# Moving a two-axis Fourier transform into the attention stage: feature axis first, chunk by chunk, and one batch's transforms beside the other batch's work

## The reference, cut to what matters

```python
# stage 1: blockwise linear attention with a decay per head
for b in range(nb):
    intra = einsum('bhic,bhjc->bhij', qb, kb) * Dmask      # lower triangle, lam**(i-j)
    out[:, :, sl] = intra @ vb + (qb * lam_pow) @ kv_state
    kv_state = lam_block * kv_state + (kb * rev_pow).T @ vb
# stage 2: Fourier mixing, layer norm, a wide MLP
u = x + real(fft(fft(x, axis=1), axis=2))                  # axis 1: tokens, axis 2: features
un = (u - mean(u)) / sqrt(var(u) + 1e-6)
x = u + relu(un @ w_ch1) @ w_ch2                           # 512 -> 2048 -> 512
# stage 3: causal convolution over 5 tokens as a gate
gate = sigmoid(sum_k conv_w[k] * x shifted)
out = (gate * (x @ w_val)) @ w_out
```

## Time and profile before

| | us |
|---|---|
| median of 3 runs | 487.25 (487.1 to 487.63) |
| the profiled execution, its own time | 487.47 |
| its span | 485.7 |
| busy: PE, DVE, POOL, ACT | 453.2, 245.2, 169.1, 135.7 |

### The profile page before, as it was taken

How to read it: one execution, slowest core, us unless ns; L and a number is a source line. 1 busy time by engine, 2 the same in 40 slices (tenths; PEclk the granted TensorE clock), 3 DMA queues, 4 the chain that set the end, 5 groups by cost and what they waited for, 6 DMA issues and landing times.

```text
span 485.7 us, 6750 instructions
## 1 busy us (share of the span) xinstructions
PE 453.2 (93%) x2700; PEld 435.9 (90%) x2700; DVE 245.2 (50%) x342; ACT 135.7 (28%) x240; POOL 169.1 (35%) x107
## 2 busy tenths in 40 slices
PE   6999998297979999999999999999999999399997
PEld 5999997296869999999999999999999999399885
DVE  2334758948986132753212321322262899799110
ACT  1252435020543106211022211112123524434221
POOL 1341978546496300520003300013106309235320
PEclk9699999598989999999999999999999999699999
DMA  7997300000202200130000220001400000001112
GB/s 227 363 372 239 103 1 0 1 1 0 87 0 88 86 1 0 43 131 1 1 0 2 86 86 0 0 0 33 142 0 1 1 1 0 0 1 65 66 43 87
DMA packets 12009, 28.69 MB, mean 59 GB/s; under 512 B 1352, under 2 KB 3024, under 8 KB 11984
## 3 DMA queue, kind: packets, MB, share of 16 engines
q1 hardware_dynamic: 11984, 28.34, 16.8%
HBM read 25.18 MB, written 3.15 MB: 58 GB/s over the span
## 4 chain that ended last, share of the span: by engine, by line
PE 76%; DVE 17%; DMA 2%; issue 2%; POOL 1%; ACT 1%; DVEq 0%
PE ps L692 8%; PE ps L693 8%; PE ps L691 8%; PE ps L669 8%; PE ps L667 8%; PE ps L668 8%; DVE xT L1145 5%; PE ps L535 5%; PE ps L507 2%; PE ps L756 2%; PE ps L757 2%; PE ps L755 2%; PE ps L518 2%; PE ps L734 2%; PE ps L735 2%; PE ps L736 2%
## 5 line engine op out<-in xcount | busy, mean ns | idle before, releaser
L1088 DVE SCALAR_TENSOR_TENSOR hl<-ps,hh 128x384 fp32r<-128x384 f32 x64 | 34.9, 555 | 123.8 <-ACT hh L842 123.6
L842 ACT ACTIVATE hh<-ps 128x384 fp32r<-128x384 f32 x64 | 31.3, 490 | 169.3 <-PE ps L669 169.3
L1228 POOL TENSOR_TENSOR w1l_a<-raw_a,w1h_a 128x1024 fp32r<-128x1024 f32 x4 | 10.0, 2498 | 120.5 <-ACT w1h_a L798 120.5
L1145 DVE SCALAR_TENSOR_TENSOR xT<-u_pad,cw,xT 128x768 f32<-128x768 f32 x32 | 44.6, 1460 | 6.0 <-ACT xT L869 6.0
L691 PE MATMUL ps<-hh,w2h_a 128*128 128x384 f32 x128 | 45.1, 352 | 0.0
L667 PE MATMUL ps<-cen_h,w1h_a 128*128 128x384 f32 x128 | 43.5, 340 | 0.2 <-issue 0.2
L692 PE MATMUL ps<-hl,w2h_a 128*128 128x384 f32 x128 | 43.4, 339 | 0.0
L693 PE MATMUL ps<-hh,w2l_a 128*128 128x384 f32 x128 | 43.4, 339 | 0.0
L669 PE MATMUL ps<-cen_h,w1l_a 128*128 128x384 f32 x128 | 43.3, 338 | 0.0
L691 PE MATMUL ps<-hh,w2h_b 128*128 128x384 f32 x128 | 43.2, 338 | 0.0
L693 PE MATMUL ps<-hh,w2l_b 128*128 128x384 f32 x128 | 43.2, 338 | 0.0
(11 more groups left out here) (167 smaller groups left out, 1028.1 us busy)
## 6 DMA issues: line engine op xcount, KB each, us to landing
chunks<-in_qkv SPq DMA_DIRECT2D x12, 512.0 KB, 5.8
chunks<-in_qkv SPq DMA_DIRECT2D x24, 256.0 KB, 6.8
raw_a<-in_mlp SPq DMA_DIRECT2D x8, 512.0 KB, 4.6
raw_b<-in_mlp SPq DMA_DIRECT2D x8, 512.0 KB, 4.5
out<-out_sb SPq DMA_DIRECT2D x12, 256.0 KB, 2.0
raw_a<-in_val SPq DMA_DIRECT2D x2, 512.0 KB, 4.4
raw_b<-in_out SPq DMA_DIRECT2D x2, 512.0 KB, 4.2
seq_c<-const_seq SPq DMA_DIRECT2D x1, 642.0 KB, 11.7
```

The costliest lines, as they stand in the source:

```text
L842: nc.scalar.activation(hh[:, slot, j], ps[2 * slot + j][:, 0:TB], ACT.Relu).then_inc(s_hh, 1)
L1088: stt(hl[:, slot, j], ps[2 * slot + j][:, 0:TB], 0.0, hh[:, slot, j].bitcast(F32), ALU.max, ALU.subtract).then_inc(s_hl, 1)
L1145: stt(xT[:, b, r], u_pad[:, b, r, PAD - d:PAD - d + S], cw[:, K - 1 - d, r:r + 1], xT[:, b, r], ALU.mult, ALU.add).then_inc(s_tap, 1)
```

## The change: what it does, and its diff

- **Attention output.** The values are now stationary and the masked scores moving, so the output comes out transposed and goes straight to `xT`: no transposes, no identity, no `x_tok`. A product has 64 stationary columns and writes the lower or the upper half of the partitions. The state product is likewise eight products of 64 x 64 instead of four of 128 x 128.
- **Banks.** The scores have two banks instead of four, so `scores(n+1)` waits until both masks of chunk n are done. The hidden blocks of the MLP have two banks instead of four as well: `hidden(n+1)` waits for `hidden_lo(n)`.
- **Transforms.** The feature axis comes first, per chunk: `radix4` on DVE (four instructions), `hid_transform` on PE, five copies on ACT. Then the radix-6 stage over the chunks of a batch on DVE (`chunk_pair`, `two_pairs`, `third_pair`: 514 columns an instruction, 16 instructions a batch), `mirror` on ACT, and `seq_tile` on PE: twelve products with at most 128 moving columns for each of four feature tiles. `add_u` now has eight DVE instructions a tile instead of four.
- **Placing.** Batch 0's radix-6 stage and tiles stand in batch 1's attention. Batch 1's stand in the first steps of the MLP on batch 0, whose step order is changed for that.
- **Memory and transfers.** The chunk buffers are a ring of three: the load of chunk n waits for the attention of chunk n-3.
- **Tail.** `x3_lo` (four instructions) and `gate_lo` (sixteen) move from POOL to DVE.

```diff
-        START_ORDER = [(0, 0), (1, 0), (2, 0), (2, 1), (3, 0), (3, 1), (0, 1), (1, 1)]
+        START_ORDER = [(0, 0), (1, 0), (0, 1), (1, 1), (2, 0), (2, 1), (3, 0), (3, 1)]
...
+            def from_chunk(n):
+                for hp in range(HP):
+                    for par in range(2):
+                        m = mm(out_bank(n)[par * Dh:(par + 1) * Dh, hp * P:(hp + 1) * P], vr[c][:, 2 * hp + par, :],
+                               probs[:, n % 2, 2 * hp + par, :], start=n % NC == 0 and hp == 0, stop=True,
+                               skip_group_check=True)
...
+            def hid_transform(n):
+                for i in range(2):
+                    mm(bank[:, cols], z[:, i], hid_c[:, cols], start=True, stop=True)
+                mm(bank[:, 2 * P:4 * P], z[:, 2], hid_c[:, 2 * P:4 * P], start=True, stop=False)
+                mm(bank[:, 2 * P:4 * P], z[:, 3], hid_c[:, 4 * P:6 * P], start=False, stop=True).then_inc(s_hy, 1)
...
+            def seq_tile(b, a):
+                t = b * R + a
+                if a == 0:
+                    pe.wait_ge(s_r6, R6 * (b + 1))
+                for im, bank in ((0, ps[COS]), (1, ps[SIN])):
+                    if t:
+                        pe.wait_ge(s_u, UA * (t - 1) + (UA if im else UA // 2))
+                    for g, (re_row, im_row) in enumerate(((4, 5), (1, 2))):
+                        mm(o, spectrum(b, re_row, im, a), seq_c[:, at:at + P], start=True, stop=False)
+                        mm(o, spectrum(b, im_row, im, a), seq_c[:, at + P:at + 2 * P], start=False, stop=True)
...
+            for n in range(N):
+                if n + 1 < N:
+                    scores(n + 1)
+                if n % NC < NC - 1:
+                    state_product(n)
+                if n % NC:
+                    from_state(n)
+                if n >= 1:
+                    hid_transform(n - 1)
+                from_chunk(n)
+                if NC + 1 <= n < NC + 1 + R:
+                    seq_tile(0, n - NC - 1)
+            hid_transform(N - 1)
             mean(0)
-            hid_transform(1, 2)
-
             mlp_hidden(first_steps[0])
-            mlp_hidden(first_steps[1])
-            mean(1)
 
             def mlp_step(st, after):
+                if after and st.n != 3:
+                    mlp_hidden(after)
+                if st.n == 1:
+                    seq_tile(1, 1)
+                if st.n == 2:
+                    seq_tile(1, 3)
+                mlp_out(st)
                 if st.n == 0:
+                    seq_tile(1, 0)
+                if st.n == 1:
+                    seq_tile(1, 2)
+                if st.n == 3:
+                    mean(1)
+                    mlp_hidden(after)
...
+            def third_pair(b):
+                chunk_pair(b, 2)
+                tt(y[:, 0], y[:, 0], sd[:, 2], ALU.add).then_inc(s_r6, 1)
+                tt(y[:, 2], sd[:, 1], sd[:, 2], ALU.subtract).then_inc(s_r6, 1)
+                tt(y[:, 5], sd[:, 4], sd[:, 5], ALU.add).then_inc(s_r6, 1)
...
             def mlp_step(st, after):
-                if after and st.n > 1:
+                if st.n == 3:
+                    add_mlp(st)
+                    for hf in range(2):
+                        centre(1, hf)
+                        cen_lo(1, hf)
+                if after:
                     hidden_lo(after)
-                add_mlp(st)
+                if st.n in (1, 2):
+                    add_u(1, 2 * (st.n - 1))
+                if st.n != 3:
+                    add_mlp(st)
                 if st.n == 0:
-                    centre(1, 1, (0,))
+                    third_pair(1)
+                if st.n in (1, 2):
+                    add_u(1, 2 * st.n - 1)
...
+                if st.n == M_LAST + 3:
+                    x3_lo(0)
                 if st.n in (M_LAST + 4, M_LAST + 6):
                     taps(0, st.n - M_LAST - 4)
+                if st.n in (M_LAST + 5, M_LAST + 6):
+                    x3_lo(st.n - M_LAST - 4)
```

More of the change, by code:

```diff
@@ L38, in fourier_constants, with hid, seq @@
     p = np.arange(P)[:, None]
[L39 to L43, removed]
+    R, G = D // P, S // P
+    def hid(k):
+        th = 2 * np.pi * ((p * k[None, :]) % D) / D
+        return np.cos(th), np.sin(th)
+    n = np.arange(P // 2)
+    c0, s0 = hid(R * n)
+    im0 = -s0
+    im0[:, :1] = hid(np.array([D // 2]))[0]
+    c2, s2 = hid(R * n + 2)
+    odd = 2 * np.arange(P) + 1
+    co, so = hid(odd)
+    turn = np.where(odd % R == 1, 1.0, -1.0)[None, :]
+    hid_tab = np.concatenate([c0, im0, c2, -s2, co, -so, -so * turn, -co * turn], 1).astype(np.float32)
+    def seq(g, count):
+        th = 2 * np.pi * ((p * (G * np.arange(count)[None, :] + g)) % S) / S
         return np.cos(th), np.sin(th)
@@ L174, in program @@
+        with ExitStack() as second_l:
+            cen_l1 = sb_in(second_l, "cen_l1", [P, R, S], F32R)
+        mirrored = sd[:, :, 0:D].rearrange("p g (i k) -> p g i k", i=2)
+        sb("region3_rest", [P, NC * YW])
         raw = [raw_a, raw_b]
@@ L760, in _ @@
             value(0)
-            for tb in range(NB):
-                if tb + 1 < NB:
-                    value(tb + 1)
-                project(tb)
+            value(1)
+            project(0)
+            value(2)
+            project(1)
+            value(3)
+            project(2)
+            project(3)
         @block.scalar
@@ L1172, in mlp_step @@
                     taps(0, st.n - M_LAST - 4)
+                if st.n in (M_LAST + 5, M_LAST + 6):
+                    x3_lo(st.n - M_LAST - 4)
             each_step(dve, mlp_step)
             finish_mlp(3, nc.vector, dve)
-            for r in range(R):
-                gated(0, r)
+            gated(0)
+            gate_lo(0)
+            x3_lo(3)
             taps(1, 0)
-            for r in range(R):
-                gated(1, r)
+            gated(1)
+            gate_lo(1)
             taps(1, 2)
@@ L1182, in _ @@
             for tb in (2, 3):
-                for r in range(R):
-                    gated(tb, r)
+                gated(tb)
+                gate_lo(tb)
         @block.gpsimd
@@ L1289, in _ @@
             split_lo(AFTER_G, value_splits())
-            x3_lo(0)
-            x3_lo(1)
-            x3_lo(2)
             split_lo(AFTER_V, out_splits())
-            gate_lo(0)
-            x3_lo(3)
-            for tb in range(1, NB):
-                gate_lo(tb)
 def kernel(**inputs):
```

793 lines of the change are left out of this document (327 added, 466 removed).

## The result

The changed kernel takes 498.76 us (median of 4 runs, 496.85 to 504.38) against 487.18 in the runs beside it: 1.023 times the time before, 95% interval 1.018 to 1.028. The prediction said 498.5. The time is right, and the mechanism is right in the main: PE gains in the attention and loses more than that in waits for DVE inside the MLP's first steps.

The account below looks back on a forecast made before the run. PE was taken to bound attention and MLP, DVE the transforms and tail. Hidden(31) ending 9.2 us later (attention gain, MLP waits, clock) and 1.8 of tail gave 487.5 + 9.2 + 1.8 = 498.5 us; range 488 to 508.

Parts of the forecast that it names:

- The chunk: Attention on PE: a chunk's five parts, transposes gone and feature transform added, take 4.98 us instead of 5.27.
- The column-half rival: Attention's chunk part: column halves take turns instead of overlapping, 0.97 us more a chunk, 505.5 us in all; chance 0.20.
- The ring of three: Chunk loads: the ring starves PE, 9 chunks by up to 0.8 us, 7 us, 505.5 us in all; chance 0.05.
- First tile of batch 0: In batch 1's attention: PE waits 5.1 us for third_pair(0), which ends at 62.1; the tile ends at 64.8.
- T: End of three turns of 4.98 + 2.65 + 0.3 us after batch 0's first tile: 88.5 us.
- The MLP's first steps: Batch 1's tiles (10.6 us) and PE's waits (19.6 us) stand inside the MLP, the longest wait 6.9 us at third_pair(1).
- The clock: Clock falls behind PE's waits of over 3 us ahead of the MLP's steady part: 3 x 2.0 = 6 us, bounds 0 and 14.
- newton: MLP step 7: newton(0) and newton(1) together on DVE make hidden_lo(9) late for hidden(10) by 1.4 us, bounds 0 and 3.
- The tail: Behind hidden(31): x3_lo on DVE ahead of gated(0), less 2.1 us of collision, 0.3 for waits: 1.8 us more.
- 1.14 us a tap alone: Tail on DVE: price of a tap without POOL working, against 2.1 us beside POOL; taps(0, 2) takes 12.8 instead of 14.92.
- The signs: Trace signs: PE idle ahead of tiles, clock 0.5 behind, hidden(5) near 181 us, L436 about 1.1, DVE busier, POOL less.
- DVE undisturbed: Rival: none of the charged DVE collisions with POOL happens, gaining 13.9 us, 484.6 us in all; chance 0.14.

Follow-up runs that it names:

- the third experiment: Against the changed kernel, the four x3_lo and sixteen gate_lo go back from DVE to POOL; 502.1 us, ratio 1.032 to the kernel before.
- fourth experiments: Against the changed kernel, hidden blocks from step 5 on use four banks in turns of two; 498.23 us, ratio 1.024 to the kernel before.
- the filled waits: Against the changed kernel, PE multiplies ones into a free bank in five waits for DVE; 497.03 us, ratio 1.021 to the kernel before.
- the first experiment: Against the changed kernel, each feature tile of batch 1 stands one MLP block later in PE's list; 485.92 us, ratio 0.998 to the kernel before.

## Why the prediction was right, and where not

- **The chunk** (4.98 us forecast, 5.13 measured). State product 0.6 and 0.61, feature transform 1.30 and 1.31, chunk's part 1.1 and 1.02. What was missed is 0.20 us on the state's part, 1.09 instead of 0.89. It now stands behind the 64-column products, and its operands have changed places (the state is stationary), which the prediction did not count among the changes. Once, behind the full-array products of a tile, the same eight records take 0.94 us from end to end (91.92 to 92.86):

```profile
91.53 0.39 PE L476 MATMUL ps<-seq_c,sd 128*128 128x64 f32 x2
91.75 1.11 PE L425 MATMUL ps<-qd,state 128*128 128x128 f32 x8
```

So most of the 0.20 us comes with the change of shape. The Trainium skill, TensorEngine Tiling (Array Packing), section Key Properties, says that a change of tiling mode drains the engine; the extra time behind the change of shape agrees.
- **The column-half rival** fell: the halves overlap. The ring of three cost no wait in mid-stream that matters (in this profile PE waited for `chunks` once, 1.29 us at the start; in others it waited up to 0.99 us ahead of `scores(8)` in turn 7, and at most 1.3 us in all, where the rival had 7), so that rival fell too.
- **First tile of batch 0**: forecast at 62.1 after a wait of 5.1 us, measured at 61.46 after 2.93; PE came later, since the products behind the wait of 3.35 us ran at a granted clock of 0.61. **T**, the end of the last tile turn: 88.5 forecast; the last tile of batch 0 ended at 91.7; the tile behind the first wait took 5.3 us at 1.2 GHz instead of 2.65.
- **The MLP's first steps**: third_pair's wait 6.9 forecast, 5.48 measured; the others 2.7, 2.2, 2.6, 0.6 and 3.7 forecast, 2.75, 2.31, 2.74, 0.84 and 3.07 measured. Here the step failed that put the first variance among the work of out(0) at no cost: the epsilon waits behind `two_pairs(1)`, 3.47 us. Since 1.4 of that shortens the next wait, the term was 2.1 us too small.
- **The clock** (6 us, bounds 0 and 14): 10.8 in the profiled execution, 7.5 and 7.7 in those of the third and fourth experiments. In the median it is about 5, an estimate: 10.8 less 5.6, if all of the profiled execution's excess is the clock's. The size stood within its bounds and near its value; the filled waits show the mechanism, not the median's size.
- **newton** (1.4 us): 1.40 measured.
- **The tail** (+1.8 us) had the wrong sign. From the last relu of hidden(31) to `gated(0)` on PE it was 24.36 us and is 22.77 (415.33 to 438.10), so -1.6. The step that failed is "1.14 us a tap alone": the 9.13 us for eight taps in the earlier trace rows had a POOL `x3_lo` beside them for 1.8 us (381.86 to 385.38), whose row was not among those read:

```profile
381.86 3.52 POOL L1253 TENSOR_TENSOR cen_l<-u_pad,cen_h 128x1536 fp32r<-128x1536 f32 x1 [5.02 <-ACT cen_h L861]
```

Alone a tap is 0.94 us. The change took that collision away together with the work that caused it: the first eight taps fell by 1.6 us and the second by 3.2, where 2.1 was forecast. The third experiment brings both collisions back.
- **Sum for the profiled execution**: hidden(31)'s relu came at 415.33 where 405.7 was forecast, 9.6 late: 4.8 of clock above the 6, 2.1 of epsilon, and the rest in the chunks and small gaps. The tail gave 3.4 back against its term, and 0.3 behind `gated(0)`: 498.5 + 9.6 - 3.4 - 0.3 = 504.4. Of this the median has 5.6 less. That the forecast met the median within 0.3 us is luck: with the clock at about 5 instead of 6, the terms that were too small (2.1 and some 2.7 of chunks and small gaps, the latter not taken apart) are offset by the tail's 3.4.
- **The signs.** DVE's busy sum rose and POOL's fell as said, L436 takes 1.02 us, and PE idles ahead of the tiles. hidden(5) was forecast near 181 us and started at 190.05, in the third experiment's profile at 186.76, so the signs held but for the place of hidden(5).
- **DVE undisturbed** (484.6) fell as a case, since its collisions are there: 2.85 us for L898. But part of it was right, in the tail.
- **What the forecast did not ask**: whether the waits belong to the change or to its order. They belong to the order. With the same work, four banks for the hidden blocks and lists sorted by need the change is worth 2.3% (476.38 against 487.0), with fillers 3.0%.

## What to carry to other kernels

Where two engines feed each other in strict lists, put at least one whole block between an instruction and the one on the other engine that waits for it; four calls moved by one block were worth 12.8 us here, and overlap without that distance was 8 to 10 us slower than the plain serial order. Sort an engine's list by who waits for each instruction: a half-microsecond instruction that frees a bank must not stand behind a stage of several microseconds. When work moves off an engine, look for what it slowed there before you price the move, and read a duration as "alone" only after looking at the other engine's row at that time.

## What the runs showed of the hardware that was not expected

- DVE and POOL: the taps lost more than half of the time that POOL worked beside them: 4.2 us for 7.5 us of weight splits (11.72 against 7.53, in the changed kernel), 3.25 for the 3.64 us of an `x3_lo` (14.97 against 11.72, in the third experiment). The Trainium skill, SBUF — State Buffer, section Who interferes with whom, says that a VectorE instruction with two SBUF inputs contends with a GpSimd instruction that reads SBUF; these rows agree. The size, 0.56 and 0.89 of POOL's time, is measured here.
- Column halves with 128 moving columns took 1.02 us for 16 records, slightly less than row halves (1.09), and 64 x 64 products 0.61 for 16 records, more than half of it.
- The falls of the clock differ from run to run of one kernel. The changed kernel's four runs spread over 7.5 us, with mean granted clocks of 0.948 to 0.964, while the first experiment, with shorter waits, spread over 2.5 us in 12 runs.
